# First group's routing spread between the search passes, its token slots one step later, and the second layer of its last slot moved into the second group's routing

## Chip, cores and metric

The program runs on one core of a Trainium2 chip. The metric is the device time of one execution in microseconds (us), lower is better.

## What is computed

Top-32 attention over 2 x 8 heads of 576 rows, then a mixture of eight experts (one expert for each token), then a dense mixture of four experts. The parts of the reference that matter:

```python
scores = scale * np.matmul(q, k.transpose(0, 1, 3, 2))
kth = np.partition(scores, -32, axis=-1)[..., -32:-31]
scores = np.where(scores >= kth, scores, -1000000000.0)      # then softmax
x = softmax(scores) @ v                                      # (1152, 512) after the heads are joined
logits = x @ w_gate + modality_bias[modality_id]
e_idx = np.argmax(logits, axis=1)                            # one expert of 8 for each token
out[mask] = gate_w[mask, None] * (np.maximum(x[mask] @ w1[e], 0.0) @ w2[e])
out2 += p[:, e:e + 1] * (np.maximum(x @ w1b[e], 0.0) @ w2b[e])   # four dense experts, all tokens
```

All of it is float32. Most products are done as three matmuls of rounded high and low parts.

## The kernel before

**Tiles and groups.** The 1152 tokens are 9 tiles of 128. A tile has 8 heads, so attention is 72 head steps (HEADS). Tiles 0 to 2 are the first group (GA), tiles 3 to 8 the second (GB). When the logits of a group are known, its tokens are sorted by expert into slots of 128 rows (at least one slot for each expert in use); each slot runs one expert's two layers. The slots of GA are worked during the attention of the later tiles, those of GB after attention. The four dense experts follow.

**Attention.** The program is one list of steps p = 0 to 77 on each engine, written out by hand. PE makes the scores of head p, multiplies attention by v for head p-6 (`att_times_v`) and transposes the attention of head p-5 (`transpose_att`). ACT copies scores, transposes and products out of PSUM and takes the exponential. POOL masks (`mask`, lines 656 and 659) heads 0 to 69, DVE the last two (line 1305). DVE finds the 32nd largest score of each row: for a pair of heads, 14 passes, that is two MAX8 on the scores (line 1093), then three rounds of two MATCH_REPLACE8 (line 1102) and two MAX8 (line 1107) (`find_thresholds`). After each pass it calls `pause()`, which takes one further piece of `work_beside` and moves DVE's clock on by 1/7 of a head.

**Routing.** `pick` finds each token's expert, `ranks` (PE) counts, `place` makes the tables: lines 1207 to 1271, about 30 small DVE instructions for GA, nine pieces between `yield`s. Inside a piece a helper `step` issues an instruction and waits for its semaphore before the next. `sum_tokens` (PE, line 1559) turns them into row numbers, by which POOL gathers the slots' rows. For GB the same pieces run in one go after attention; there the last tile is counted apart (`more_ranks`, lines 1551 and 1553, one tile at a time).

**GA's slots.** PE works slot s at steps A_START + 7s: `a_up` (first layer, line 1576), `a_turn` (transposes of the hidden values), `a_down` (second layer, line 1592), which reads `w2_raw`. Five slots (SPREAD) are in the list, from step 40; the fifth's second layer is at steps 73 and 74. SP loads weights (`a_load1`, `a_load2`), stores (`a_store`).

**First expert of GB.** Its number is known early (`turn_experts`, `spread_first` at step FIRST_AT = 66). SP loads its w1 into `w1_early`; ACT rounds it (`early_high`), POOL subtracts (`early_low`, line 672) at heads 67 to 70. Its w2 goes into `w2_raw` (`first_down`) after GA's fifth slot; ACT (`split_high`, line 885) and DVE (`split_low`, line 1279) split it.

**End of attention.** Step 77: the last two single counts, transposes of six heads of x (`x_most_transposes`), the last `att_times_v`; then `last_logits`, `pick_last`, `place(GB)`, `sum_tokens`, gather, `turn_slot(0)` (transpose of the gathered rows, line 1434), the register loads of the number of slots, `slot(0)`. A GB slot is 24 matmuls of layer one, three groups of four transposes, 24 matmuls of layer two (lines 1439 to 1441). After the last one DVE splits the first dense expert's w1 and copies the last slot's result (`copy_y`, line 1336), for which PE waits before `up_first`.

Each engine runs its own list in order. A wait holds everything behind it on that engine.

## Time and profile before

| | us |
|---|---|
| median of 3 runs | 920.28 (919.24 to 922.7) |
| the profiled execution | 921.51 |
| its span in the trace | 919.8 |

| engine | busy, us | share of the span |
|---|---|---|
| PE (matmul) | 860.4 | 94% |
| PE weight load | 724.1 | 79% |
| DVE | 551.2 | 60% |
| ACT | 341.1 | 37% |
| POOL | 295.5 | 32% |

The shares are means over stages with different limits. Times in the views are microseconds from the start of the span; a timeline row gives start, duration, engine, line of the kernel, operation, output and input, count, and in brackets the idle time ahead of it with what ended it. DVE is full to about 384 us, PE from about 417 us; between lies the end of attention and the second group's routing.

### The profile page before, as it was taken

Reading aid. Unit: us, or ns where it says so; the run is one execution under the profiler, and the core shown is the slowest. Engines: PE = TensorE matmul, PEld = TensorE weight load, DVE = VectorE, ACT = ScalarE, POOL = GpSimd, SP = SyncE. Lnnn points to the kernel's source line nnn. Section 1 sums busy time; section 2 is a strip of 40 time slices with the busy share of each in tenths; the row PEclk is TensorE's granted clock in tenths of the full one; section 3 lists DMA queues with packets and bytes.
Section 4 is the critical chain, followed back from the end, with each engine's and each line's share of the span. In section 5 each row is a group of like instructions: output and inputs, shape, how many; then the busy total and the mean of one; then the engine's idle time right before and its main releaser. Section 6 shows DMA issues by size and latency. Waiting matters only on the chain.

```text
span 919.8 us, 13596 instructions
## 1 busy us (share of the span) xinstructions
PE 860.4 (94%) x4895; PEld 724.1 (79%) x4895; DVE 551.2 (60%) x1087; ACT 341.1 (37%) x726; POOL 295.5 (32%) x243
## 2 busy tenths in 40 slices
PE   6799999948899999858999899999999999999998
PEld 5688888835566676646787789989898999899896
DVE  5999999999999999833482523414132422332121
ACT  5455556525465665431472412203130311222010
POOL 7876677547687666711110200000000000000000
PEclk9599999979899999868999999999999999999999
DMA  9320000024254355046193600112002200000001
GB/s 208 92 92 23 14 12 13 13 96 165 78 201 137 128 184 206 12 141 251 35 341 106 229 36 1 50 42 92 1 1 92 91 0 0 0 0 0 34 16 52
DMA packets 49394, 75.60 MB, mean 82 GB/s; under 512 B 24624, under 2 KB 24624, under 8 KB 49328
## 3 DMA queue, kind: packets, MB, share of 16 engines
q1 hardware_dynamic: 43088, 60.62, 19.4%
q0 software_dynamic: 4160, 13.63, 4.7%
q10 hardware_dynamic: 2080, 0.52, 0.3%
q8 instruction: 35, 0.57, 0.2%
q14 instruction: 31, 0.25, 0.1%
HBM read 63.49 MB, written 11.27 MB: 81 GB/s over the span
## 4 chain that ended last, share of the span: by engine, by line
PE 57%; DVE 38%; issue 4%; DMA 1%; ACT 1%; SPq 0%; DVEq 0%; POOLq 0%; ACTq 0%
PE bank L1439 17%; PE bank L1441 17%; PE bank L1440 17%; DVE work L1102 17%; DVE top L1107 13%; DVE top L1093 5%; PE bank L1434 2%; PE bank L1592 1%; PE bank L1495 1%; DMA k_raw<-in_k_dram 0%; DMA b_xs_raw<-x_dram,b_tok_i 0%; DVE b_hsTl L1349 0%; DVE kTl L1054 0%; PE bank L1466 0%; ACT b_hsTh L980 0%
## 5 line engine op out<-in xcount | busy, mean ns | idle before, releaser
L1107 DVE MAX8 top<-work 128x8 f32<-128x576 f32 x216 | 152.2, 743 | 0.1
L656 POOL TENSOR_SCALAR att<-sc,top 128x576 f32<-128x576 f32 x70 | 120.7, 1724 | 93.2 <-DVE top L1107 93.0
L1439 PE MATMUL bank<-xT,w1h 128*128 128x384 f32 x384 | 129.4, 337 | 3.4 <-DVE b_ys L1336 3.4
L1376 DVE SCALAR_TENSOR_TENSOR hT<-bank,hT 128x384 fp32r<-128x384 f32 x96 | 52.8, 557 | 131.0 <-ACT hT L1005 124.2
L1441 PE MATMUL bank<-xT,w1h 128*128 128x384 f32 x384 | 128.9, 336 | 0.0
L1440 PE MATMUL bank<-xT,w1l 128*128 128x384 f32 x384 | 128.9, 336 | 0.0
L1005 ACT ACTIVATE hT<-bank 128x384 fp32r<-128x384 f32 x96 | 46.9, 491 | 198.7 <-PE bank L1441 195.5
L1439 PE MATMUL bank<-w2h,hT 128*128 128x512 f32 x288 | 112.2, 390 | 1.2 <-DVE hT L1376 1.2
L1441 PE MATMUL bank<-w2l,hT 128*128 128x512 f32 x288 | 112.2, 390 | 0.0
L1440 PE MATMUL bank<-w2h,hT 128*128 128x512 f32 x288 | 112.2, 389 | 0.0
L1102 DVE MATCH_REPLACE8 work<-top,work 128x576 f32<-128x576 f32 x144 | 106.7, 746 | 0.0
L659 POOL TENSOR_TENSOR att<-att,ex 128x576 f32<-128x576 f32 x70 | 99.0, 1414 | 5.8
L1495 PE MATMUL bank<-v_one,attT 128*128 128x65 f32 (+1 forms) x800 | 93.3, 274 | 1.5 <-ACT av L805 1.3
L1495 PEld LDWEIGHTS bank<-v_one,attT 128*128 128x128 f32 (+1 forms) x800 | 85.9, 188 | 10.6 <-issue 7.2
L1388 DVE SCALAR_TENSOR_TENSOR x_tok<-bank,pr_e,x_tok 128x512 f32<-128x512 f32 x27 | 20.3, 751 | 115.0 <-PE bank L1441 115.0
L1439 PEld LDWEIGHTS bank<-xT,w1h 128*128 128x128 f32 x384 | 72.6, 189 | 4.1 <-issue 3.8
L1440 PEld LDWEIGHTS bank<-xT,w1l 128*128 128x128 f32 x384 | 72.6, 189 | 0.3
L1441 PEld LDWEIGHTS bank<-xT,w1h 128*128 128x128 f32 x384 | 72.5, 189 | 0.0
L797 ACT ACTIVATE attT<-bank 128x512 f32<-128x512 f32 x72 | 43.0, 597 | 79.7 <-PE bank L1466 78.0
L1605 PE MATMUL bank<-v_one 128*128 128x260 f32 x270 | 67.4, 397 | 0.0
L782 ACT ACTIVATE sc<-bank 128x576 f32<-128x576 f32 x72 | 46.4, 644 | 53.1 <-PE bank L1484 52.7
L1439 PEld LDWEIGHTS bank<-w2h,hT 128*128 128x128 f32 x288 | 54.1, 188 | 12.5 <-DVE hT L1376 1.5
(272 smaller groups left out, 1431.9 us busy)
## 6 DMA issues: line engine op xcount, KB each, us to landing
w_raw<-in_moe_w_dram SPq DMA_DIRECT2D x92, 512.0 KB, 6.0
q_raw<-in_q_dram SPq DMA_DIRECT2D x18, 128.0 KB, 2.9
v_one<-in_v_dram POOLq DMA_DIRECT2D x18, 128.0 KB, 4.9
out_dram<-x_tok SPq DMA_DIRECT2D x9, 256.0 KB, 2.0
y_dram<-zero POOLq DMA_DIRECT2D x2, 1024.0 KB, 6.7
w_early<-in_moe_w_dram SPq DMA_DIRECT2D x4, 512.0 KB
y_dram<-b_ys POOLq DMA_DIRECT2D x7, 256.0 KB, 2.6
k_raw<-in_k_dram SPq DMA_DIRECT2D x6, 256.0 KB, 4.8
```

The lines of the kernel that those rows point to most:

```text
L656: nc.gpsimd.tensor_scalar(att[:, g % ATR, :], sc[:, g % RING, :], top8[:, g % RING, 3, 7:8], None, ALU.is_ge).then_inc(keep_made, 1)
L659: nc.gpsimd.tensor_tensor(att[:, g % ATR, :], att[:, g % ATR, :], ex[:, g % EXR, :], ALU.mult).then_inc(att_made, 1)
L782: nc.scalar.activation(sc[:, g % RING:g % RING + 2, cols], bank[:, SB:SB + 2, 0:HS], ACT.Copy, scale=float(D) ** -0.5).then_inc(sc_copied, 1)
L1005: nc.scalar.activation(hTh(b)[:, f, :], bank[:, HB + f % 4, 0:BW], ACT.Relu).then_inc(h_high, 1)
L1102: nc.vector.match_replace(out=work[:, j, :], in_to_replace=top8[:, g % RING, i, :], in_values=sc[:, g % RING, :] if i == 0 else work[:, j, ...
L1107: nxt = nc.vector.max(out=top8[:, g % RING, i + 1, :], in_=work[:, j, :])
L1376: nc.vector.scalar_tensor_tensor(out=hTl(b)[:, f, :], in0=bank[:, HB + f % 4, 0:BW], scalar=0.0, in1=f32(hTh(b)[:, f, :]), op0=ALU.max, op ...
L1439: nc.tensor.matmul(dst, high_lhs, high_rhs, start=start, stop=False)
L1440: nc.tensor.matmul(dst, low_lhs, high_rhs, start=False, stop=False)
L1441: return nc.tensor.matmul(dst, high_lhs, low_rhs, start=False, stop=stop)
L1495: last = nc.tensor.matmul(bank[r0:r1, AVB, 0:W], attT[:, g % 2, c, r0:r1], v_one[b][:, h, c, :], start=(c == 0), stop=(c == KC - 1))
L1605: nc.tensor.matmul(bank[:, bk, 0:(KC - 1) * W], still[:, 0:P], moving, start=True, stop=True)
```

## The change

1. **GA's `place`** is cut into single instructions (or two that don't depend on each other) between the passes; `settle()` waits for the step before, one pass later. For GA the two int32 tables come straight from the reduction, without casts. A_START goes from 40 to 41, TOKENS_AT from 38 to 39. SP's first weight load no longer waits for the table.
2. **First expert of GB** is found ten steps earlier (from tile 3 alone); its `early_high` goes with slot 3 instead of 4, its `early_low` to heads 62, 63, 65, 66. `pick` for tiles 4 to 7 is one call between the two parts of the last division.
3. **End of attention:** the last head uses other PSUM banks (`head_banks`), so its transposes run ahead of the product of the head before; tile 7's transposes and logits are a step later; GB's counts go behind `last_logits` in one group, the last tile's in its own tensor `hot_last`.
4. **Second layer of GA's fifth slot:** its halves go behind `last_ranks` and behind `sum_tokens`. With it go ACT's `a_copy_y(4)` and SP's `a_store(4)`. `w2` for GB's first slot is loaded in two halves, each behind the half that frees `w2_raw`, and split in two halves, the second inside slot 0.
5. **GB slots:** the number of slots is loaded ahead of `turn_slot(0)`. In `slot` the transposes of the first hidden half go into the second half of layer one. At the end PE waits for the last `copy_y` behind `up_first`; DVE copies between the halves of the split.

```diff
-        RANKS_AT, TOKENS_AT, A_START, A_STEP, SPREAD = 36, 38, 40, 7, 5
+        RANKS_AT, TOKENS_AT, A_START, A_STEP, SPREAD = 36, 39, 41, 7, 5
-            ... p == t * H + (18, 18, 17, 22, 22, 22, 22, 17)[t]
+            ... p == t * H + (18, 18, 17, 22, 22, 22, 22, 18)[t]
-        FIRST_AT = HEADS - 6
+        FIRST_AT = HEADS - 16
+        EARLY = (62, 63, 65, 66)
+        def head_banks(g):
+            return (MB, SB + 1) if g == HEADS - 1 else (TBK, AVB)
 # SP
-                yield from clock.until(A_START + A_STEP * SPREAD)
-                a_store(SPREAD - 1)
+                yield from clock.until(1000)
+                keep_x(T - 1)
                 with sp.If(guarded(sp, GA, SPREAD)):
                     sp.sem_inc(passed, 1)
                 with sp.Else():
+                    sp.wait_ge(a_half_d, 1)
+                    first_down((0, 1))
                     sp.wait_ge(a_d, SPREAD)
-                    first_down()
-                yield from clock.until(1000)
-                keep_x(T - 1)
+                    first_down((2, 3))
+                a_store(SPREAD - 1)
 # POOL
-                if g >= HEADS - 1 - DC:
-                    early_low(g - HEADS + 1 + DC)
+                if g in EARLY:
+                    early_low(EARLY.index(g))
-            early_low(DC - 1)
 # ACT
-                yield from clock.until(A_START + A_STEP * SPREAD)
+                yield from clock.until(1000)
                 a_copy_y(SPREAD - 1)
...
-                if s >= 1:
-                    act.wait_ge(slot_y, s)
-                for i in range(2):
+                    if i == 0 and s >= 1:
+                        act.wait_ge(slot_y, s)
+                    if i == 1:
+                        slot_xT(s + 1)
                     act.wait_ge(slot_hT, 2 * s + i + 1)
-            split_high(0, w2_raw, w2h, w2_loaded, w2_high)
+            split_high(0, w2_raw, w2h, w2_loaded, w2_high, (0, 1))
             slot_xT(0)
 # DVE, place(): each step(...) becomes go(g, ...), yield, settle()
+                def settle():
+                    dve.wait_ge(g.route_step, g.steps)
-                step(nc.vector.tensor_scalar(g.counts[:, 1, :], total, 0.0, None, ALU.is_gt))
+                go(g, nc.vector.tensor_scalar(g.counts[:, 1, :], total, 0.0, None, ALU.is_gt))
+                yield
+                settle()
...
+                    if g is GA:
+                        with nc.allow_low_precision(reason="whole numbers below 100"):
+                            nc.vector.tensor_reduce(out=g.table_i[:, :, :], in_=g.cmp_pre[:, :, :, :], axis=AX.X, op=ALU.add).then_inc(g.experts_made, 1)
-                yield from place(GA, 1, clock.until(TOKENS_AT - 3.4))
-                yield from clock.until(FIRST_AT - 3)
-                yield from pick(GB, 0, GB.tiles - 3, 1)
+                yield from place(GA, 1, clock.until(TOKENS_AT - 2))
+                yield from clock.until(FIRST_AT - 5)
+                yield from pick(GB, 0, 1, 1)
             def last_slot(s):
-                split_low(ke, w1_raw, w1h, w1l, w1_high, w1_split)
+                split_low(ke, w1_raw, w1h, w1l, w1_high, w1_split, (0, 1))
                 copy_y(s - 1)
+                split_low(ke, w1_raw, w1h, w1l, w1_high, w1_split, (2, 3))
 # PE
+                    if s + 1 == SPREAD:
+                        break
                     yield from clock.until(at + 5)
                     a_down(s, (0, 1, 2, 3))
...
                 yield from clock.until(1000)
+                a_down(SPREAD - 1, (0, 1, 2, 3))
+                yield from clock.until(1001)
+                a_down(SPREAD - 1, (4, 5, 6, 7))
+                        if i == 1 and c == 2:
+                            if s >= 1:
+                                pe.wait_ge(slot_hT_split, 2 * s)
+                            turn_hidden(0)
...
             last_logits()
-            more_ranks(GB, GB.tiles - 1, 3)
+            pe.wait_ge(sc_copied, HEADS)
+            ranks(GB)
+            last_ranks()
+            clock.now = 1000
+            advance(work_beside)
             sum_tokens(GB)
-            clock.now = 1000
+            clock.now = 1001
             for _ in work_beside:
                 pass
-            turn_slot(0)
             pe.wait_ge(GB.table_made, 2)
...
+            turn_slot(0)
...
             pe.wait_ge(slot_hT_split, slots * 2)
-            pe.wait_ge(slot_y_copied, slots)
...
             up_first()
+            pe.wait_ge(slot_y_copied, slots)
```

## Rows read from the trace of the kernel before

**Rows 1.** Windows of all engines: start:end, length, busy us (PE PEld DVE ACT POOL), PE clock, DMA share, GB/s
```profile
350.00:371.00 21.00, 21.00 (x137) 14.89 (x136) 21.00 (x46) 13.17 (x31) 14.40 (x9) 1.00 0.62 226
376.00:383.00 7.00, 7.00 (x19) 3.89 (x19) 7.00 (x15) 3.27 (x8) 6.92 (x4) 0.62 0.01 2
416.60:422.30 5.70, 5.70 (x13) 4.45 (x14) 3.02 (x3) 0.18 (x1) 0.44 (x1) 0.50 1.01 390
514.70:517.80 3.10, 3.09 (x10) 3.09 (x11) 3.10 (x4) 0.57 (x1) 0.43 (x1) 0.50 0.83 251
```

**Rows 2.** The page: shares of the chain that ended last
```profile
PE 57%; DVE 38%; issue 4%; DMA 1%; ACT 1%; SPq 0%; DVEq 0%; POOLq 0%; ACTq 0%
```

**Rows 3.** Timeline of DVE, 185 to 200 us, first group's routing
```profile
185.29 0.74 DVE L1107 MAX8 top<-work 128x8 f32<-128x576 f32 x1
...
188.07 1.30 DVE L1217 CAST a_table_i<-a_table 128x18 int32<-128x18 f32 x1
...
197.02 0.17 DVE L1259 CAST a_by_slot_i<-a_by_slot 128x10 int32<-128x10 f32 x1
197.10 0.75 DVE L1107 MAX8 top<-work 128x8 f32<-128x576 f32 x1
...
199.32 0.09 DVE L1102 MATCH_VALUE_LOAD work<-top,work 128x8 f32 x1
```

**Rows 4.** Timeline of POOL in the same stretch
```profile
187.94 1.40 POOL L659 TENSOR_TENSOR att<-att,ex 128x576 f32<-128x576 f32 x1
```

**Rows 5.** Timeline of DVE, 383 to 399 us, end of attention
```profile
383.58 3.00 DVE L1305 SCALAR_TENSOR_TENSOR att<-sc,top,ex 128x576 f32<-128x576 f32 x1
386.79 0.82 DVE L1305 SCALAR_TENSOR_TENSOR att<-sc,top,ex 128x576 f32<-128x576 f32 x1 [0.21 <-DVE att L1305]
387.53 0.17 DVE L1160 TENSOR_TENSOR logits<-logits,bias_t 128x16 f32<-128x16 f32 x1
387.73 0.17 DVE L1161 TENSOR_REDUCE b_lmax<-logits 128x2 f32<-128x16 f32 x1
...
398.64 0.29 DVE L1135 TENSOR_TENSOR x_cur<-av,rden 128x128 f32<-128x128 f32 x1
```

**Rows 6.** Timeline of PE, 373 to 391 us
```profile
373.95 0.66 PE L1434 MATMUL bank<-ident,x_cur 128*128 128x128 f32 x4 [2.67 <-DVE x_cur L1135]
374.44 1.97 PE L1495 MATMUL bank<-v_one,attT 128*128 128x65 f32 x9
...
377.49 5.51 PE L1592 MATMUL bank<-w_raw,hsT 128*128 128x512 f32 x8
...
386.82 3.68 PE L1592 MATMUL bank<-w_raw,hsT 128*128 128x512 f32 x8
390.34 1.23 PE L1495 MATMUL bank<-v_one,attT 128*128 128x65 f32 x10
```

**Rows 7.** Timeline of POOL at the end of its masks
```profile
381.30 4.66 POOL L672 TENSOR_TENSOR w1l<-w_early,w1h 128x1024 fp32r<-128x1024 f32 x2
```

**Rows 8.** Timeline of PE, 406 to 417 us, second group's routing
```profile
406.51 1.45 PE L1559 MATMUL bank<-b_slot_token,b_row_hot 128*128 128x14 f32 x6 [4.08 <-DVE b_row_hot L1246]
...
412.61 1.12 PE L1434 MATMUL bank<-ident,b_xs_raw 128*128 128x128 f32 x4 [4.66 <-DMA b_xs_raw<-x_dram,b_tok_i]
...
416.60 0.79 PE L1439 MATMUL bank<-w1h,b_xsTh 128*128 128x512 f32 x1 [2.87 <-issue]
```

**Rows 9.** Timelines of PE in the second slot, then of ACT in the fifth
```profile
440.00 0.50 PE L1439 MATMUL bank<-w2h,b_hsTh 128*128 128x512 f32 x1 [0.57 <-DVE b_hsTl L1349]
...
475.38 1.06 ACT L885 ACTIVATE w2h<-w_raw 128x1024 fp32r<-128x1024 f32 x1 [0.17 <-DMA w_raw<-in_moe_w_dram]
```

**Rows 10.** Timeline of all engines between the slots and the dense experts
```profile
509.04 4.63 DVE L1279 TENSOR_TENSOR w1l<-w_raw,w1h 128x1024 fp32r<-128x1024 f32 x4 [2.31 <-ACT w1h L885]
...
513.58 0.68 DVE L1336 COPY b_ys<-bank 128x512 f32<-128x512 f32 x1
...
514.71 0.68 PE L1439 MATMUL bank<-xT,w1h 128*128 128x384 f32 x1 [3.38 <-DVE b_ys L1336]
```

More of the change, by code:

```diff
@@ L151, in routing_tensors @@
             g.cmp_slot = temps.take(f"{nm}_cmp_slot", [P, s, E])
+        hot_last = consts.take("hot_last", [P, E])
         routing_tensors(GA, consts)
@@ L484, in a_store, with load @@
                 sp.dma_start(y_a[s * P:(s + 1) * P, :], ys[:, :]).then_inc(a_stored, 16)
-            def load(e, kth, raw, src, split, loaded):
+            def load(e, kth, raw, src, split, loaded, parts=range(DC)):
                 sp.wait_ge(split, kth * DC + BASE)
@@ L489, in load @@
                 n = raw.shape[1] // DC
-                for c in range(DC):
+                for c in parts:
                     sp.dma_start(raw[:, c * n:(c + 1) * n, :], rows[:, c * n:(c + 1) * n, :]).then_inc(loaded[c], 16)
@@ L1208, in place @@
                                               jcol[:, 0:n].rearrange("p (o j) -> p o j", o=1).broadcast_to([P, E, n]), ALU.is_gt))
-                step(nc.vector.tensor_scalar(g.counts[:, 1, :], total, 0.0, None, ALU.is_gt))
-                step(nc.vector.tensor_reduce(out=g.counts[:, 0, :], in_=g.cmp_cnt[:, :, :], axis=AX.X, op=ALU.add))
-                step(nc.vector.tensor_tensor(g.cmp_pre[:, :, :, :], below[:, :, :].rearrange("p (o e) f -> p o e f", o=1).broadcast_to([P, 2, E + 1, E]),
+                go(g, nc.vector.tensor_scalar(g.counts[:, 1, :], total, 0.0, None, ALU.is_gt))
@@ L1212, in place @@
+                yield
+                settle()
+                go(g, nc.vector.tensor_reduce(out=g.counts[:, 0, :], in_=g.cmp_cnt[:, :, :], axis=AX.X, op=ALU.add))
+                yield
+                settle()
+                go(g, nc.vector.tensor_tensor(g.cmp_pre[:, :, :, :], below[:, :, :].rearrange("p (o e) f -> p o e f", o=1).broadcast_to([P, 2, E + 1, E]),
                                              g.counts[:, :, :].rearrange("p c (o f) -> p c o f", o=1).broadcast_to([P, 2, E + 1, E]), ALU.mult))
@@ L1222, in place @@
                 if g is GA:
-                    experts()
-                    nc.vector.tensor_copy(g.kth_expert_i[:, :], g.kth_expert[:, :]).then_inc(g.experts_made, 1)
+                    yield from experts()
                 yield
-                step(nc.vector.scalar_tensor_tensor(out=g.lg_a2[:, :, :], in0=over_t(g.table[:, 0, 0:E], n), scalar=float(P), in1=before_it, op0=ALU.mult, op1=ALU.add))
-                step(nc.vector.tensor_tensor(g.lg_a2[:, :, :], g.lg_a2[:, :, :], g.onehot[:, 0:n, :], ALU.mult))
@@ L1228, in place @@
-                step(nc.vector.tensor_reduce(out=g.pos_f[:, :], in_=g.lg_a2[:, :, :], axis=AX.X, op=ALU.add))
+                go(g, nc.vector.scalar_tensor_tensor(out=g.lg_a2[:, :, :], in0=over_t(g.table[:, 0, 0:E], n), scalar=float(P), in1=before_it, op0=ALU.mult, op1=ALU.add))
                 yield
+                settle()
+                go(g, nc.vector.tensor_tensor(g.lg_a2[:, :, :], g.lg_a2[:, :, :], g.onehot[:, 0:n, :], ALU.mult))
+                yield
+                settle()
+                go(g, nc.vector.tensor_reduce(out=g.pos_f[:, :], in_=g.lg_a2[:, :, :], axis=AX.X, op=ALU.add))
@@ L1316, in _ @@
             pick_last(GB)
-            for _ in place(GB, 4):
+            for _ in place(GB, 2):
                 pass
@@ L1546, in ranks, with last_ranks @@
                 last.then_inc(g.rank_made, 1)
-            def more_ranks(g, t, part):
-                n, rows = g.tiles, bank[:, g.rank_bank, :]
-                pe.wait_ge(g.hot_made, part)
-                nc.tensor.matmul(rows[:, t * E:(t + 1) * E], before[:, :], g.onehot[:, t, :], start=False, stop=False)
-                for u in range(t + 1, n + 1):
-                    last = nc.tensor.matmul(rows[:, u * E:(u + 1) * E], ones[:, :], g.onehot[:, t, :], start=False, stop=(t == n - 1))
-                last.then_inc(g.rank_made, 1)
+            def last_ranks():
+                n, rows = GB.tiles, bank[:, GB.rank_bank, :]
+                pe.wait_ge(GB.hot_made, 3)
+                nc.tensor.matmul(rows[:, (n - 1) * E:n * E], before[:, :], hot_last[:, :], start=False, stop=False)
+                nc.tensor.matmul(rows[:, n * E:(n + 1) * E], ones[:, :], hot_last[:, :], start=False, stop=True).then_inc(GB.rank_made, 1)
             def sum_tokens(g):
@@ L1685, in slot @@
                     last.then_inc(slot_h, 1)
-                if s >= 1:
-                    pe.wait_ge(slot_hT_split, 2 * s)
-                for i in range(2):
-                    pe.wait_ge(slot_relu, 2 * s + i + 1)
-                    transposes(HTB + i, lambda c: b_hs[:, (4 * i + c) * P:(4 * i + c + 1) * P]).then_inc(slot_hT, 1)
-                    if i == 0:
-                        turn_slot(s + 1)
+                turn_slot(s + 1)
+                turn_hidden(1)
                 if GA.tiles <= s < 2 * GA.tiles:
```

171 lines of the change are left out of this document (110 added, 61 removed).

## Prediction, made before the changed kernel was run

> **What bounds the kernel now.** I read the chain that ended last first: 38% of it is DVE and 57% PE [rows 2]. Then windows by stage: to 371 us DVE is busy in all of each window, and PE as well at the full clock [rows 1]. DVE sets the pace there, since its search passes follow each other without idle time, and the scores of the last pair were copied at 367.6 us, while DVE came to them at 373.8, so PE has some 6 us in hand. From the end of the search at 383.6 [rows 5] to the first GB slot at 416.60 [rows 8], 33 us, neither engine is full: the heads still in the pipeline, and the second group's routing. From 416.60 on PE is full but for short waits. So three kinds of time count: DVE time before 383, the chain of waits from 383 to 416, and holes of PE after it.
>
> **1. GA's routing on DVE.** From 185.29 to 199.32 are 14.03 us [rows 3]; in it lie six MAX8 at 0.66 us start to start and three MATCH_REPLACE8 with their value load at 0.72, together 6.1. The routing's 30 instructions take the other 7.9 us. An instruction that waits for the one before starts 0.20 us after it (387.53, then 387.73, duration 0.17) [rows 5]; one that doesn't wait starts 0.08 after (197.02, then 197.10, duration 0.17) [rows 3]. So a wait costs 0.12, and 19 of the steps lose theirs: 2.3 us. The other part is what POOL costs. The cast at 188.07 took 1.30 us instead of 0.17 and ended as POOL's multiply of 187.94 to 189.34 ended [rows 3, 4]; with four smaller ones I count 2.0 us of such waits in the 7.9. That cast becomes a reduction. But now the instructions lie over three pairs in which POOL masks steadily, not in a clump at which POOL ran dry: before, 17 small instructions beside a busy POOL lost 2.9 us, and without the cast's 1.1 that is 0.10 each, 2.9 for 30. So 2.3 + 2.0 - 2.9 = 1.4, and the two casts that go give 0.3: **1.7 us**. Bounds: 4.3 without any POOL wait; -3 if each waits twice as long as I take.
>
> The Trainium skill (SBUF — State Buffer, "SBUF: two separate sides") says that the read and write ports which DVE and GpSimd share are locked for a whole instruction, also against a DVE instruction with two SBUF inputs. By that rule spreading is a cost, and its reductions are safe. The cast row agrees; the third of POOL's time spent on two-input multiplies times 17 exposed instructions at 0.7 us gives an estimate of 4 us instead of 2.9, and the term would be 0.6.
>
> Tokens now come at DVE's step 37, so POOL waits with mask 35 for about 3 us. PE's first slot is a step later and PE has 6 us in hand; nothing is added.
>
> **2. End of attention.** The attention of head 70 took 3.00 us on DVE against 0.82 for head 71 [rows 5], while POOL ran its last two subtractions of w1 (381.30 to 385.96) [rows 7]. These now run at heads 62 to 66: 2.2 us less, head 71 is masked at 385.4 instead of 387.6. Before, PE then had a half of the second layer ahead of it (386.82, 3.68 us) and only at 390.34 took up head 69's product [rows 6]; the other half at 377.49 took 5.51 us at the low clock (1.2 GHz; mean 0.62 of the stretch) [rows 1, 6]. After, head 69's product is done by 381.7, and behind head 70's transposes at 384.45 come: transposes, tile 7's logits, head 71's transposes, product of 70, three transposes of x, product of 71. The product takes 1.23 us at the full clock and 1.97 at the low one [rows 6]. PE waits some 3 us before this, and before a wait of 2.67 us was followed by the low clock [rows 6]. So I take low: 1.1 + 1.2 + 1.1 + 2.0 + 0.8 + 2.0 = 8.2, ending at 392.65; a copy and three small DVE steps make x whole at 393.65. Before it was whole at 398.93 [rows 5]. **5.3 us**; with the sum at the full clock (5.2) 8.3.
>
> **3. Second group's routing.** GB's counts (14 matmuls, 1.5 us) move behind the last logits, beside DVE's `pick_last` of 1 us: tables start 0.75 us later against x. So `row_hot` is ready at 406.5 - 4.55 = 401.9. In front of `sum_tokens` stands now the first half of the second layer, from 397.9; at the low clock it takes 5.3 us, to 403.2. Sum to 404.6 (before 407.96 [rows 8]), so the lead is 3.3. The second half takes 3.7 (clock up again by then, as before at 383 after 6 us of dense work [rows 1, 6]) to 408.3. Behind it stand a branch with its register load (1.1) and two register loads: three took 2.87 us ahead of 416.60 [rows 8], so 1.9: PE is free at 411.3. The gather starts at 405.8 and took 3.5 us, to 409.3, or 1 more beside the load of w2. Now ACT: it copies y at 408.4, branches, then rounds w2's first half, loaded from 403.7 (2 x 512 KB, by 410), at 1.04 us each [rows 9], to 412.05, and only then the slot's rows (0.6); DVE 0.7: **slot 0 starts at 413.4 instead of 416.60**. Of 5.3 us 3.2 are left, so this part costs 2.1. Cheapest: the loads of the registers hidden and no second layer in the way, a gain of 1.4 more. Dearest: w2's half lands after 9.6 us (the slowest weight load in the trace), ACT has it at 415.9 and slot 0 starts at 417.2, a loss of 5.9. Queued behind the wait for the second layer: on ACT the rounding and the slot's rows, on SP the second half of w2 and y's store, on POOL three gathers of x, all needed by 420 at the earliest.
>
> The first layer of slot 0 still runs 5.7 us at half clock [rows 1].
>
> **4. In the slots.** Before, PE waits 0.57 us ahead of the second layer [rows 9]. After, only the second hidden half is awaited, with `turn_slot` beside it: 0.3 less in four slots, 1.2 together. But where an expert changes, ACT is busy with w2: its last chunk ends at 476.4 [rows 9], then the relu takes 0.6, to 476.95, while PE now wants it at 475.85 in the middle of layer one; a loss of 1.0 there and 0.5 in the slot before, 0.1 in the sixth. Net **-0.4**, between -1.6 and 1.2.
>
> **5. Slots to dense.** PE waited 3.38 us, for DVE's `copy_y` behind the whole split of w1 [rows 10], and then ran 3.1 us at half clock [rows 1]. Now the first chunk (split at 510.3) is all it needs, and PE makes 2.05 us of matmuls from each chunk of 1.15. **3.4 us**. If PE too needs time for the branch, as DVE with 2.31 idle [rows 10], 1.1; if the clock stays up, 3.1 x 0.5 = 1.5 more, 4.9.
>
> The rest has one answer: w1 of the first expert arrives a good 20 us before its use, its rounding finds ACT at 60% busy, `hot_last` and the banks add one copy of 0.2 us that hides beside the counts.
>
> **Sum.** 1.7 + 5.3 - 2.1 - 0.4 + 3.4 = 7.9 us. The profiled execution would go from 921.5 to 913.6. It was 1.2 above the median of the three runs; on the median's scale 920.3 - 7.9 = **912.4 us**.
>
> **Rivals.**
> - *The clock stays up.* Dense work at 397.9 to 408 and fewer holes could keep PE at 2.4 GHz: 3.0 more in part 2, and slot 0's first layer without 5.7 us at half clock, 2.9 more. 920.3 - 13.8 = 906.5. For it: the hole of part 5 goes. Against: PE waits again some 5 us ahead of slot 0, as before [rows 1, 8].
> - *Waits on DVE are free.* The 0.12 is then no cost of the wait but of the operand, and part 1 is 2.3 less: 914.7. The Trainium skill says so (VectorE: DVE Perf Modes, "The DRAIN you can't avoid"): a semaphore after each of eight copies cost nothing. The spacings 0.20 and 0.08 speak against it here [rows 3, 5].
> - *The second layer is only moved.* It fills no hole, but lengthens the chain to slot 0: low clock in both halves (5.3 + 5.3) and w2's half late. Slot 0 at 417.2, part 3 costs 5.9: 916.2.
> - *Slower: the port.* Each spread instruction waits for POOL. The price is up to 1.13 us [rows 3]; 17 exposed ones make 19 us, part 1 is -15 and the time 929. It decides from 0.6 us on each exposed one, when part 1 eats the other 6.2. Against it: of 17 instructions before only two waited over half a microsecond.
>
> **How the numbers follow.** Forecast 0.45; clock up 0.2; waits free 0.1; only moved 0.15; port 0.05; something that I don't see 0.05. The range from **905.5 to 917.5** takes in the first four with the bounds of part 4 and 5 and leaves out the port and half of the rest. A measurement of this kernel can tell 0.5% (4.6 us) from no change: faster is below 915.7, which holds the forecast, the clock and waits free, mostly, and a third of only moved: 0.77. Same 0.17, slower 0.06.
>
> **What would show it.** Part 1: from the first routing instruction of GA to the last some 38 us instead of 13, but the pair (70, 71) starts at about 372 instead of 373.8. Part 2: att of head 70 in 0.82 us; x whole about 10 us after the last search pass instead of 15.4; clock 0.5 there. Part 3: the L1592 groups at about 396 and 403 (with part 1's gain), `sum_tokens` directly behind the first, ACT's rounding as the last thing ahead of slot 0. Part 4: a PE wait in the middle of layer one in slots 3 and 4. Part 5: no wait at L1439 behind the last slot. I am wrong if the last pair starts later than 373.8, if the lead at slot 0 is under 2 us or above 8, or if a new wait shows between the slots.

## The result, and the profile after

| | before | after |
|---|---|---|
| median, us | 921.21 (5 runs, 919.24 to 924.39) | 914.49 (5 runs, 913.67 to 915.15) |
| profiled execution, us | 921.51 | 913.67 |
| its span, us | 919.8 | 911.9 |

The ratio of after to before is 0.9931, interval 0.9906 to 0.9956: the change gives 6.7 us, where 7.9 were forecast. The two profiled executions differ by 7.9 us of span, but 2.3 of these belong to neither kernel: the first search pass began at 14.35 us after and at 16.63 before, because the first scores came sooner, and the same start varies between 14.2 and 16.6 us among the runs of this study (15.96 in e7, which is the kernel before up to there). I therefore compare stages, each from its own beginning (read from the timelines of DVE and PE). The search is DVE's passes for the thresholds and ends with its last MAX8. x is whole when DVE has written the last part of `x_cur`. Slot 0 starts with its first matmul of layer one, and the dense experts with their first:

| stage, us | before | after | gain | forecast |
|---|---|---|---|---|
| pair 32 to pair 38 (GA's routing) | 39.21 | 36.52 | 2.7 | |
| pair 38 to the end of the search | 169.46 | 171.15 | -1.7 | |
| both | 208.67 | 207.67 | 1.0 | 1.7 |
| end of the search to x whole | 15.38 | 10.64 | 4.7 | 5.3 |
| x whole to slot 0 | 17.67 | 21.89 | -4.2 | -2.1 |
| slot 0 to the dense experts | 98.11 | 95.44 | 2.7 | 3.0 |
| dense experts to the end | 405.04 | 403.65 | 1.4 | 0 |
| sum | | | 5.6 | 7.9 |

The windows of the kernel after, as in [rows 1] (start:end, length, busy us of PE PEld DVE ACT POOL, PE clock, DMA share, GB/s). The third is new, the first half of the moved second layer with the counts before it:

```profile
350.00:371.00 21.00, 20.62 (x118) 13.52 (x116) 21.00 (x43) 11.16 (x31) 18.77 (x12) 1.00 0.35 113
376.00:383.00 7.00, 4.72 (x24) 4.36 (x24) 5.91 (x11) 1.99 (x6) 0.00 (x0) 0.61 0.01 2
396.00:400.40 4.40, 4.40 (x9) 2.33 (x9) 3.37 (x15) 0.00 (x0) 0.00 (x0) 0.50 0.00 0
412.81:418.50 5.69, 5.69 (x13) 4.47 (x14) 2.21 (x2) 0.16 (x1) 1.96 (x3) 0.50 0.37 118
508.20:511.30 3.10, 3.05 (x17) 3.05 (x18) 3.10 (x4) 3.10 (x4) 0.57 (x1) 1.00 0.22 90
```

DVE is still full to the end of the search. Slot 0's first layer still starts at half clock (fourth row), and the first dense matmuls now run at the full clock (fifth row; 0.50 in [rows 1]). The chain that ended last, which was [rows 2], now runs over PE for most of the span:

```profile
PE 70%; DVE 21%; POOL 3%; issue 2%; ACT 2%; DMA 1%; SPq 0%; DVEq 0%; ACTq 0%; POOLq 0%
```

**DVE in the search.** The timeline of DVE after, answering [rows 3], then where the second group's first expert is named, ten heads earlier than before:

```profile
187.08 0.28 DVE L1241 TENSOR_REDUCE a_table_i<-a_cmp_pre 128x18 int32<-128x144 f32 x1
187.29 0.61 DVE L1244 TENSOR_TENSOR a_cmp_kth<-a_table,ecol 128x64 f32<-128x64 f32 x1
...
198.75 1.00 DVE L1308 TENSOR_SCALAR a_by_slot_i<-a_by_slot 128x10 int32<-128x10 f32 x1
...
299.10 0.17 DVE L1194 TENSOR_SCALAR turned_by<-turned_less 128x8 f32<-128x8 f32 x1
299.30 1.26 DVE L1195 TENSOR_TENSOR turned_less<-turned_less,turned_by 128x8 f32<-128x8 f32 x1
```

POOL's timeline at the same place:

```profile
299.12 1.42 POOL L670 TENSOR_TENSOR att<-att,ex 128x576 f32<-128x576 f32 x1
```

The cast of 1.30 us is a reduction of 0.28. But an instruction on 128x8 took 1.26 us and ended as POOL's mask ended (300.56 and 300.54), as the cast did in [rows 3, 4]. From pair 46 to 60 the kernel after needs 71.86 us and the one before 67.77; later it gets 2.4 of these back (60.44 and 62.85 us to the end; 62.15 in e7, so 1.7 to 2.4), where the pieces stood before.

**From the search to slot 0.** DVE, to set beside [rows 5]:

```profile
380.31 0.82 DVE L1365 SCALAR_TENSOR_TENSOR att<-sc,top,ex 128x576 f32<-128x576 f32 x1
...
390.63 0.29 DVE L1146 TENSOR_TENSOR x_cur<-av,rden 128x128 f32<-128x128 f32 x1
```

PE, to set beside [rows 6, 8]:

```profile
377.70 2.37 PE L1563 MATMUL bank<-v_one,attT 128*128 128x65 f32 x10 [1.07 <-ACT av L816]
381.28 0.44 PE L1531 MATMUL bank<-ident,att 128*128 128x128 f32 x1 [1.21 <-DVE att L1365]
...
393.11 2.69 PE L1613 MATMUL bank<-b_onehot,ones 128*128 128x48 f32 x12
...
396.51 6.12 PE L1658 MATMUL bank<-w_raw,hsT 128*128 128x512 f32 x8
402.06 1.13 PE L1625 MATMUL bank<-b_slot_token,b_row_hot 128*128 128x14 f32 x6
403.05 3.68 PE L1658 MATMUL bank<-w_raw,hsT 128*128 128x512 f32 x8
410.74 0.66 PE L1497 MATMUL bank<-ident,b_xs_raw 128*128 128x128 f32 x4 [4.02 <-DMA b_xs_raw<-x_dram,b_tok_i]
412.81 0.80 PE L1502 MATMUL bank<-w1h,b_xsTh 128*128 128x512 f32 x1 [1.41 <-DVE b_xsTl L1382]
```

ACT and POOL in the same stretch:

```profile
408.17 2.00 ACT L896 ACTIVATE w2h<-w_raw 128x1024 fp32r<-128x1024 f32 x2 [0.81 <-issue]
411.44 0.60 ACT L971 ACTIVATE b_xsTh<-bank 128x512 fp32r<-128x512 f32 x1 [1.27 <-PE bank L1497]
```

```profile
404.32 1.05 POOL L728 DMA_INDIRECT b_xs_raw<-x_dram,b_tok_i  x1 [28.56 <-DVE b_pos_i L1272]
```

The attention of head 70 takes 0.82 us as forecast. The last thing ahead of slot 0 is not ACT's rounding (done at 410.17) but the gather: issued at 404.32, its rows reach PE at 410.74. That is 6.42 us, where the kernel before needed 3.5.

**Slots and dense.** PE in slot 3, and at the join that [rows 10] showed with 3.38 us of waiting:

```profile
459.00 0.63 PE L1497 MATMUL bank<-ident,b_hs 128*128 128x128 f32 x4 [0.49 <-ACT b_hs L985]
...
508.25 0.44 PE L1502 MATMUL bank<-xT,w1h 128*128 128x384 f32 x1 [0.18 <-issue]
```

### The profile page after: what moved, and what is told of

Same layout as the page of the kernel before. It is cut to its first block, busy times and chain, and to the rows that moved or that the text cites. A ratio compares the mean times of both kernels' runs of the same rounds, so it can differ in the third digit from the quotient of the medians.

```text
span 911.9 us, 13566 instructions
## 1 busy us (share of the span) xinstructions
PE 862.8 (95%) x4885; PEld 725.5 (80%) x4885; DVE 550.0 (60%) x1087; ACT 341.7 (37%) x726; POOL 296.4 (33%) x243
## 4 chain that ended last, share of the span: by engine, by line
PE 70%; DVE 21%; POOL 3%; issue 2%; ACT 2%; DMA 1%; SPq 0%; DVEq 0%; ACTq 0%; POOLq 0%
PE bank L1502 17%; PE bank L1504 17%; PE bank L1503 17%; DVE work L1113 10%; DVE top L1118 7%; PE bank L1673 6%; PE bank L1563 5%; DVE top L1104 3%; PE bank L1551 2%; PE bank L1497 2%; PE bank L1533 2%; POOL v_one L628 1%; ACT w2h L896 1%; DMA b_xs_raw<-x_dram,b_tok_i 1%; PE bank L1658 1%
## 5 line engine op out<-in xcount | busy, mean ns | idle before, releaser
L1563 PE MATMUL bank<-v_one,attT 128*128 128x65 f32 (+1 forms) x800 | 96.3, 281 | 2.2 <-ACT av L816 2.1
L1563 PEld LDWEIGHTS bank<-v_one,attT 128*128 128x128 f32 (+1 forms) x800 | 88.8, 195 | 11.8 <-issue 7.7
```

The costliest lines, as they stand in the source:

```text
L1563: last = nc.tensor.matmul(bank[r0:r1, sums, 0:W], attT[:, g % 2, c, r0:r1], v_one[b][:, h, c, :], start=(c == 0), stop=(c == KC - 1))
```

## Experiments

My theory was the sum on record. Open were: what a wait on DVE costs and what POOL does to the spread instructions; what the clock does in the drain, that is while the last heads pass through the pipeline; which wait ends last ahead of slot 0; and whether the new order inside the slots pays. A time of one execution says little: the ten of e7 lie within 5.7 us and the six of e9 within 2.3. So I compare stages. They too come from one execution each and mostly repeat within 0.1 us, but not always. Programs that are alike up to there differ by 0.6 us from pair 32 to 38 (35.94 in e11 and 35.95 in e9, 36.5 in the others), by 0.7 from pair 32 to the end of the search (208.67 before, 208.00 in e7), and by 1.2 from x whole to slot 0 (20.82 to 22.07 in after, e1, e2, e8, e11). A smaller difference in these stages shows nothing.

### The waits of the first group's routing

`e1_wait_at_once`: each wait stands directly behind its instruction again, one instruction for each pass as in the change. `e2_clumped`: the same, and several instructions in one gap between passes, in groups much as before.

```diff
                 go(g, nc.vector.tensor_scalar(g.counts[:, 1, :], total, 0.0, None, ALU.is_gt))
-                yield
                 settle()
+                yield            # e2: left out but for four places
```

> The changed kernel with one thing turned round: in GA's routing on DVE each instruction is still put alone between two search passes, but its wait stands directly behind it and not behind the next search pass. Same places, same instructions. Read from the start of the pair of heads 32 to the start of pair 38 (36.52 us after, 39.21 before). If a wait costs 0.12 us each: 19 of them, so 36.5 + 2.3 = 38.8. If waits on DVE are free (the rival): 36.5. In the whole time 2 us more or none.

> The changed kernel with GA's routing put back into its old pieces (nine, each with a wait behind every step); the two casts stay reductions and the token slots stay a step later. Pair 32 to pair 38: if the waits are the whole gain of part 1, 38.8 as in the run with waits at once. If spreading exposes the instructions to POOL as I took it (0.10 each), the pieces meet it less: 37.5 to 38.3. If the gain came from the pieces themselves, 39 or more.

Measured from pair 32 to 38: before 39.21, e2 38.95, e1 37.81, after 36.52 us. The rest of the search is untouched (46 to 60 is 71.84 and 71.85). So the gain of 2.7 splits into 0.26 for the casts (too little to be told from none), 1.14 for the spreading alone, and 1.29 for the waits, 0.07 each. There are 18 of them in `place(GA)`, not 19. A wait is not free. The 0.07 is a net value: the small instructions of this stretch last 8.95 us in all in e1 and 9.65 after, so POOL held them 0.7 us less in e1, and a wait by itself may cost up to 0.11. The part that I took for a cost, the spreading, is a gain (the small instructions last 10.31 us in e2): in e2's clump POOL's masks still met instructions, for one this row of DVE in e2 (the same instruction takes 0.18 us after):

```profile
189.19 1.02 DVE L1270 TENSOR_TENSOR a_cmp_row<-a_pos_f,jcol 128x33 f32<-128x33 f32 x1
```

### The second group's first expert off POOL's masks

`e3_off_the_masks` moves both its pieces a little later, to where POOL waits for the next thresholds; `e10_naming_alone` and `e11_pick_alone` move one each.

```diff
-                yield from clock.until(FIRST_AT)
+                yield from clock.until(FIRST_AT + 1.55)
-                yield from clock.until(FIRST_AT - 5)
+                yield from clock.until(FIRST_AT - 4.7)
```

> The changed kernel with the two pieces of DVE work that find GB's first expert moved by a few search passes, into the stretch of a pair in which POOL has finished its masks: the pick of tile 3 from DVE's step 51 to 51.3, the naming from 56 to 57.55. In the changed kernel these pieces lengthen their pairs by 1.33 and 2.76 us, 4.09 together. If POOL's masks cause the excess (each instruction takes 0.17 when alone): 2.1 together, the end of the search 2 us earlier. If it has another cause (the wait for PE's or ACT's word): 4.1 as before.

> Only one of the two moves: the naming of the second group's first expert 1.55 heads later, its pick stays where it is. The stretch from pair 46 to pair 60 should be 1.5 us shorter (of the 2.05 of both), 70.4. The clock tells two theories apart. If the clock falls in the drain because DVE's search is late against the heads, this one has most of that gain and stays at 1.00 to 384 us, with x whole 6.7 us after the search. If it was chance, it may as well be 0.50 from 378 us on, with x whole after 10.6.

> Only the other move: the pick for the second group's first expert 0.3 of a head later, its naming stays. Pair 46 to 60: 0.5 us shorter, 71.3. Clock: theory 'late search' says 0.50 from about 378 us and x whole 10.6 us after the search, as in the changed kernel, since nearly nothing is gained; theory 'chance' allows either.

| | after | e3 | e10 | e11 |
|---|---|---|---|---|
| pair 46 to 60, us | 71.86 | 69.81 | 70.08 | 71.55 |
| pair 32 to the end of the search | 207.67 | 206.78 | 207.18 | 206.79 |
| end of the search to x whole | 10.64 | 6.69 | 6.68 | 10.65 |
| one execution, us | 914.49 (median) | 906.97 | 907.58 | 914.20 |

e11's 206.79 holds 0.6 us gained in pairs 32 to 38, which its edit does not touch. DVE's naming in e10, with the instruction that took 1.26 us at 299.30:

```profile
306.53 0.17 DVE L1194 TENSOR_SCALAR turned_by<-turned_less 128x8 f32<-128x8 f32 x1
306.74 0.17 DVE L1195 TENSOR_TENSOR turned_less<-turned_less,turned_by 128x8 f32<-128x8 f32 x1
```

So 2.05 us of part 1 were lost to POOL's masks in these two places. In e3 only 0.9 of them, in e10 0.5 of 1.8, arrive at the end of the search, since DVE now waits for scores. Its timeline in e10:

```profile
328.52 1.42 DVE L1104 MAX8 top<-sc 128x8 f32<-128x576 f32 x2 [0.53 <-ACT sc L792]
...
339.30 1.42 DVE L1104 MAX8 top<-sc 128x8 f32<-128x576 f32 x2 [1.04 <-ACT sc L792]
```

The kernel after has no wait of DVE there. The larger gain was one that e3 did not aim at: PE kept the full clock through the drain, and x is whole 4 us sooner. Windows of PE in e10:

```profile
376.00:380.00 4.00, 2.74 (x24) 1.00 0.00 0
380.00:384.00 4.00, 4.00 (x39) 1.00 0.02 4
```

PE's timeline shows the other difference. In e10 PE is held at 302 us by the naming, which it hadn't waited for:

```profile
306.32 1.09 PE L1497 MATMUL bank<-ident,q_high 128*128 128x128 f32 x4 [3.96 <-DVE first_less L1190]
```

From there to the end of attention its heads run later, which I take to be what made DVE wait for the scores: head 67's product starts at 373.85 us in e10 and at 371.25 after. So the wait of 1.21 us ahead of head 70's transposes (381.28, above) does not occur. Holding PE also costs clock where it is held: the low stretch there lasts 6.8 us in e10 (305.9 to 312.7) and 3.4 after (312.7 to 316.1).

### Is it PE's lateness?

`e12_one_more_wait` takes the changed kernel and adds one wait on PE. DVE's list stays as it is.

```diff
+                if p == FIRST_AT + 1:
+                    pe.wait_ge(top_step, 5 * FIRST_AT + 6)
                 if high is not None:
                     q_transposes(high, "qh")
```

> The changed kernel with nothing but one wait more on PE: at step 57, ahead of a group of transposes, PE waits until DVE has made the second round of replacements of pair 56 (about 306.2 us), as it waits for DVE's naming at 306.3 in the kernel with the naming alone. DVE's list is untouched, so pair 46 to 60 stays 71.9 and the end of the search stays at 207.7 after pair 32. My theory of why the clock stayed up with the late naming: PE was held 4 us at 302, so its heads ran about 2.3 us later to the end and the waits ahead of head 70's transposes (1.1 to 1.2 us of them) closed; then the same happens here: PE at 1.00 to 384 us, x whole 6.7 us after the search instead of 10.6, slot 0 20.5 us behind it instead of 21.9, in all 5 us less, 909.5, by a wait that was added. The rival says that it is DVE's gained time (the search ends earlier against PE's work of the slots) and not PE's lateness: then PE is at 0.50 from 378 us on, x whole comes after 10.6, and the time is 914.5 or up to 1 us more.

I put it too early in PE's list: PE came to it at 294 us instead of 302 and stood for 13.5 us, which then starved the search (pair 46 to 60 80.04 us instead of 71.86). The time, 918.92 us (10 runs, ratio to before 0.9988, 0.9967 to 1.0009), is no gain. The rival is answered all the same, since the search here lost 9.3 us and gained nothing, and yet the clock stayed up in the profiled execution. The other nine executions had mean granted clocks of 0.954 to 0.957 against 0.959 in the profiled one, so it is not shown that they kept it too. PE's wait, then two windows around the end of the search (391.4):

```profile
307.90 2.39 PE L1563 MATMUL bank<-v_one,attT 128*128 128x65 f32 x10 [13.50 <-DVE work L1113]
```

```profile
387.50:391.50 4.00, 2.75 (x24) 2.33 (x23) 3.96 (x9) 3.80 (x11) 0.00 (x0) 1.00 0.00 0
391.50:395.50 4.00, 4.00 (x38) 4.00 (x39) 2.79 (x7) 2.00 (x7) 0.00 (x0) 1.00 0.01 4
```

x whole came 6.67 us after the search. The profiles built on the changed kernel without fillers fall into two groups. Where PE also waits ahead of head 70's transposes (1.2 to 2.3 us, beside earlier waits of 0.63, 0.19 and 1.07), the clock is 0.50 in the whole of 384 to 388 and x whole takes 10.6 us (after, e1, e2, e4, e5, e8, e11). Where it doesn't, the clock is 1.00 until x is whole and that takes 6.7 (e3, e9, e10, e12).

But this wait cannot be what lowered the clock in all of the first group. In the kernel after it lasts from 380.07 to 381.28, and the clock had fallen at 377.53. Windows of PE after:

```profile
375.00:377.50 2.50, 1.54 (x13) 1.00 0.00 0
377.70:380.00 2.30, 2.30 (x10) 0.50 0.00 0
```

In e2, e4 and e5 too the fall comes before this wait. In e1, e8 and e11 it comes 0.2 to 1.7 us after its start, as in these windows of e8 (its wait began at 379.27):

```profile
376.90:380.90 4.00, 1.30 (x11) 1.00 0.00 0
381.10:385.00 3.90, 3.46 (x17) 0.50 0.02 4
```

So the wait marks the profiles in which PE was early, and which part of PE's idle time in 370 to 381 us lowered the clock was not separated. What is shown is that the same two waits of 0.63 and 1.07 us went with a fall in some profiles and not in others, and that PE later against the search went with none.

### Filling the hole

`e6_filled` keeps PE busy in it with 24 unread matmuls (128x128).

```diff
+                if p == AV_END - 2:
+                    unread(MB + 2, 18)
                 if 0 <= p - TR_LAG < HEADS and p != AV_END - 1:
                     transpose_att(p - TR_LAG)
+                if p == AV_END - 3:
+                    pe.wait_ge(a_ys, SPREAD - 1)
+                    unread(MB + 2, 6)
```

> The changed kernel with 24 matmuls of 128 columns whose result nobody reads put into PE's two waits at the end of attention (6 ahead of head 69's product, 18 behind it), 2.6 us of work at the full clock. In the changed kernel the clock falls at 377.7 and stays at 1.2 GHz until 403. If PE's idle time there is the cause: the clock stays at 2.4 GHz through the last heads, x is whole 3 us earlier (10.6 us behind the last search pass becomes 7.6), the 14 count matmuls take 1.6 instead of 3.0 us, the first half of the second layer 3.7 instead of 5.6; slot 0 starts 3 to 6 us earlier. If the chain there is bound by ACT's and DVE's copies: x is whole at most 1 us earlier.

Measured: 910.99 us, one execution; clock 1.00 from 370 to 388. So with the two waits filled the clock did not fall. (PE was also 1.4 us later in this execution before the first filler: head 67's product starts at 372.68 instead of 371.25. In e11, where PE stood about as late, the clock fell.) x whole comes 9.17 us after the search: 1.5 less than after, and 2.5 more than in e10, which is what the fillers themselves delay. They took 1.5 and 4.2 us where I had reckoned 2.6 in all, and PE comes to head 70's transposes 2.6 us later against the search than after. The rest of the expectation failed: the clock fell again at 390.75, so the counts still took 3.6 us and the half of the second layer 5.0. x whole to slot 0 takes 20.81 instead of 21.89, which is within what this stage varies by.

### Ahead of slot 0

`e4_sum_first` puts `sum_tokens` ahead of the first half of the second layer. `e5_gather_first` keeps the order of PE, but SP loads the second layer of slot 0 only when the slot's rows have landed, and ACT rounds those rows first.

```diff
# e4, PE
+            sum_tokens(GB)
             clock.now = 1000
             advance(work_beside)
-            sum_tokens(GB)
# e5, SP, then ACT
+                    sp.wait_ge(slot_loaded[0], 16)
                     sp.wait_ge(a_half_d, 1)
-            split_high(0, w2_raw, w2h, w2_loaded, w2_high, (0, 1))
             slot_xT(0)
+            split_high(0, w2_raw, w2h, w2_loaded, w2_high, (0, 1))
```

> The changed kernel with both halves of the second layer of GA's fifth slot behind the sum of the tokens instead of one half ahead of it. In the changed kernel the first half ends at 402.1 and the sum waits for it, though DVE's table was ready at 400.7. If the half ahead is what makes the gather late: sum 1.4 us earlier, gather issued at 402.9 (on the scale of the changed kernel's trace) instead of 404.3; but w2's first half is loaded 3 us later, behind the gather, so the gather lands after 3.5 us instead of 6.4, and ACT has w2 rounded only at about 414: slot 0 starts 1 to 2 us later than 412.8. If w2 is not what ACT waits for: slot 0 up to 4 us earlier.

> The changed kernel with SP's load of w2 held back until the first gathered rows have landed, and with ACT taking slot 0's rows before it rounds w2. In the changed kernel the gather took 6.4 us from issue to landing beside the load of w2, before 3.5 us alone. If the load beside it is the cause: 3.5 us again, slot 0 starts 2.5 to 3 us earlier than 412.8, and its second layer waits for w2 at most 1 us. If the gather is slow for another reason (x stored late, the queue): 6 us as now, and no gain.

| | before | after | e4 | e5 |
|---|---|---|---|---|
| x whole to the gather's issue, us | 10.16 | 13.40 | 12.38 | 13.42 |
| issue to PE's transposes of the rows | 3.52 | 6.42 | 8.75 | 4.40 |
| x whole to slot 0 | 17.67 | 21.89 | 24.28 | 19.88 |

PE, then ACT in e4:

```profile
402.12 8.47 PE L1658 MATMUL bank<-w_raw,hsT 128*128 128x512 f32 x16
412.15 0.66 PE L1497 MATMUL bank<-ident,b_xs_raw 128*128 128x128 f32 x4 [1.55 <-issue]
```

```profile
413.94 0.58 ACT L971 ACTIVATE b_xsTh<-bank 128x512 fp32r<-128x512 f32 x1
```

In e4 the gather is issued 1.0 us sooner, but the whole second layer (8.47 us) then stands on PE between it and its use, and ACT has the result of that layer and w2 to do ahead of the rows: 2.4 us worse. In e5 the gather needs 4.40 instead of 6.42 us and slot 0 starts 2.0 us sooner; the rounding of w2 starts at 414.99, in the shade of layer one, and the gain is still there at the dense experts (x whole to dense 115.10 against 117.33). How much of the 4.2 us the loads beside the gather cost is known roughly: with the loads beside it the same gather took 4.75 (e6) to 6.4 us in nine profiles, held back 4.40 (e5) and 4.71 (e9). From x whole to slot 0, e5 is 0.9 to 2.2 us below after, e1, e2, e8 and e11, and e9 1.6 to 2.3 below e3, e10 and e12, where the clock was up as well. So holding back the loads gives some 1 to 2 us.

### The last part alone, and the old order in the slots

`e7_last_part_alone` is the kernel before with part 5 of the change only; `e8_old_slots` is the changed kernel with the old order of transposes in `slot`.

```diff
# e7, PE
-            pe.wait_ge(slot_y_copied, slots)
             up_first()
+            pe.wait_ge(slot_y_copied, slots)
# e7, DVE
-                split_low(ke, w1_raw, w1h, w1l, w1_high, w1_split)
+                split_low(ke, w1_raw, w1h, w1l, w1_high, w1_split, (0, 1))
                 copy_y(s - 1)
+                split_low(ke, w1_raw, w1h, w1l, w1_high, w1_split, (2, 3))
# e8, PE
-                        if i == 1 and c == 2:
-                            turn_hidden(0)
...
+                turn_hidden(0)
                 turn_slot(s + 1)
                 turn_hidden(1)
```

> The kernel before with one piece of the change alone: PE waits for the last slot's copied result behind the first dense layer and not ahead of it, and DVE makes that copy between the halves of the split of w1. Before, PE waited 3.38 us here and then ran 3.1 us at half clock. Expected: no wait at L1439 behind the last slot, the clock stays at full, 3.4 + 1.4 = 4.8 us less, 915.5 to 916.5, ratio 0.995. If PE also pays for leaving the nest of branches, as DVE does with 2.3 us: 1.1 less only. If the time is given back later (w2's split is not earlier): nothing.

> The changed kernel with the old order inside a GB slot: both groups of hidden transposes behind the first layer, ACT and PE as before. In the changed kernel the seven slots take 95.26 us from the first matmul of slot 0 to the last of slot 6, before 94.57. If the group in the middle of the first layer costs where an expert changes (slots 3 and 4, 0.5 and 1.0 us by my sum) and gives 0.3 elsewhere: 94.6 to 95.0 here. If the slots are longer for another reason (w2 in two halves): 95.3 still.

e7: 915.04 us (10 runs; ratio to before 0.9947, 0.9925 to 0.9969). Slot 0 to dense 94.01 instead of 98.11, dense to the end 403.65 instead of 405.04. This small part of the change gives 4.9 us (2.9 to 6.9 by the interval) where the whole gives 6.7. Its window behind the slots:

```profile
510.00:513.00 3.00, 3.00 (x19) 3.00 (x18) 3.00 (x4) 3.00 (x4) 0.57 (x1) 1.00 0.21 87
```

e8: 912.76 us, one execution; slot 0 to dense 94.59 instead of 95.44, all stages up to x whole as after. This difference by itself proves little, since the stage holds the end of a low clock of changing length and takes 94.83 to 95.66 in profiles with the same order (e10, e12). I therefore take half of the time at low clock off the length of the seven slots (first matmul of slot 0 to the last of slot 6), an estimate from the clock's two levels. With the old order this leaves 91.9 us before (94.73 with 5.69 at low clock; not 94.57, as the expectation has it), and 91.8 in e7, e8 and e9. With the new order it leaves 92.3 to 92.5 in eight profiles, among them after (95.26 with 5.68), 92.8 in e6 and 93.1 in e5. The groups do not overlap: the new order costs some 0.6 us. Only 0.1 of it is waiting: PE's idle times in the seven slots add up to 2.98 us after and 2.88 before. The rest lies in PE's busy time, and its cause was not separated.

### Three together

`e9_three_together` has the edits of e3, e5 and e8.

> The changed kernel with three edits together: the second group's first expert found a little later, beside POOL's subtractions instead of its masks; the gather of slot 0's rows ahead of the rounding and of the load of its second layer; the old order inside the slots. Single edits gave, against the changed kernel: 0.9 us less to the end of the search and 4.0 less from there to x whole (full clock); 2.0 less from x whole to slot 0; 0.5 to 0.85 less from slot 0 to the dense experts. Theory 'they add, and the clock stays up because of the late expert': 914.5 - 0.9 - 4.0 - 1.4 - 0.7 = 907.5, all runs within 1.5 us of one another. Theory 'the clock was luck of that one execution': 914.5 - 0.9 - 1.4 - 0.7 = 911.5, with PE at 0.50 from about 378 us in the profile; if it is luck in each execution, times scattered over the 4 us between. Rival, nothing adds (each gain only moves the wait to another engine): 913 or more.

903.72 us (6 runs, 902.92 to 905.2; ratio to before 0.9831, 0.9804 to 0.9858). That is 10.8 us below the changed kernel and below both theories; the executions lie within 2.3 us, and all have a mean granted clock of 0.962 to 0.964, so the clock was no luck of one execution. Against after, by stages: search 1.1 (0.6 of it in pairs 32 to 38, which no edit touches), to x whole 3.9, to slot 0 3.4, slot 0 to dense 2.0 less. Of the 3.8 us below the 907.5, 2.0 are e5's, which I had left out of the sum, and 1.3 came between slot 0 and the dense experts, where 0.7 was counted: the low clock lasts 3.4 us there instead of 5.7. PE and then a window of slot 0's start:

```profile
402.38 0.66 PE L1499 MATMUL bank<-ident,b_xs_raw 128*128 128x128 f32 x4 [2.31 <-DMA b_xs_raw<-x_dram,b_tok_i]
```

```profile
404.44:408.40 3.96, 3.96 (x10) 3.12 (x11) 0.24 (x1) 1.15 (x2) 0.00 (x0) 0.57 0.97 310
```

PE waits 2.31 us instead of 4.02 for the rows, and its half clock in slot 0 ends 3.9 us after the slot's start instead of 5.7.

## Why the prediction was right, and where its steps were off

**Part 1** (forecast 1.7, measured 1.0, or 0.3 with e7's search in place of that of the kernel before). The term of GA's routing was 1.7 and measured 2.7, and two of its parts were wrong in opposite directions. The wait was priced at 0.12 by the spacings of [rows 3, 5] and cost 0.07 net (e1), for 18 waits instead of 19. The spreading was booked as 0.9 lost to POOL and gained 1.1 (e2 against e1). What I put under "the rest has one answer", naming the second group's first expert earlier, cost 1.7 to 2.4 net: the row of 1.26 us shows an instruction held by a POOL mask, and e3 takes 2.05 us of it away by moving the pieces out of the masks. So [rows 3, 4] held the warning, and I applied it to the wrong group of instructions. The rival *waits on DVE are free* falls by e1: 1.29 us for 18 waits, twice what the stage varies by in the same program. The rule of the Trainium skill behind it (VectorE: DVE Perf Modes, "The DRAIN you can't avoid") says of a semaphore behind each of eight copies that it costs nothing; for the small instructions here e1 disagrees with 0.07 us for each. The rival *the port* is real in single places (1.26 and 1.00 us above) but not for each spread instruction.

**Part 2** (5.3, measured 4.7). The low clock was right, and the attention of head 70 is 0.82 us as worked out. The other branch was undersized: 3.0 more was forecast for a clock that stays up, e10 and e12 show 4.0. I gave that branch 0.2 and argued for the low clock by a wait of some 3 us ahead of head 70's transposes. That wait is 1.2 us, and the clock had fallen 2.5 us before it began, so the level was right and its reason was not; what lowered it stays open within PE's idle time of 370 to 381 us.

**Part 3** (-2.1, measured -4.2). Two terms were mis-sized. GB's counts were taken at 1.5 us and take 4.0 at the low clock (392.67 to 396.65; the trace has 18, not 14), so `row_hot` came 9.75 us after x whole instead of 8.25. The gather was taken at 3.5, or 1 more beside w2, and took 6.4, of which e5 and e9 put some 1 to 2 down to the load beside it. So the path was wrong as well: it was to run over ACT's rounding of w2, and it ran over the gather. Against these, the register loads, counted at 1.9, stood in the shade of the gather and cost nothing, and w2's rounding was done 1.3 us before ACT had rows to round. The halves of the second layer started at 396.51 and 403.05, close to the 396 and 403 on record, but by luck: the search began 2.3 us earlier in this trace, and counted from x whole they came at 5.6 and 12.1 us instead of 4.3 and 11.0. *The second layer is only moved* put slot 0 23.6 us behind x whole and the forecast 19.8; 21.89 lies half way, but the mechanism of that rival, low clock in both halves and w2's half too late, did not occur (the second half took 3.68 us).

**Part 4** (-0.4, measured -0.5 in the profiled pair; -0.6 by the slots of all profiles). Four waits of 0.56 to 0.61 us ahead of the second layer became 0.25, the 0.3 less of the forecast, and the waits in the middle of layer one show where they were expected, at a change of expert (459.00, 0.49 us). But all waits together changed by 0.1 us and not by 0.4, and some 0.5 us more of busy PE, for which the sum had no term, makes up the number. The size was right partly by luck.

**Part 5** (3.4, measured 3.2 and 1.4 more). The wait went, and so did the half clock behind it, which I had at 1.5 as the upper bound. With no hole in front of it there was no fall: the 4.9 of the other branch was the better value, and e7 measures it.

Together 5.6 in the profiled pair and 6.7 between the medians against 7.9; the 1.1 between the two is not explained. The total is closer than its parts: part 5 gave back 1.2 of the 3.5 that parts 1 to 4 were over. One of the prediction's own signs of being wrong came true, a lead at slot 0 under 2 us. The traces differ there by 3.8 us (416.60 and 412.81), but 2.3 of these are the earlier start, and parts 1 to 3 leave 1.5 of the 4.9 forecast. The measured 914.49 is also next to the 914.7 of *waits on DVE are free*, whose mechanism e1 refutes; the time alone could not have told them apart.

## What to carry to other kernels

Price a small instruction on DVE by what POOL does at the same moment, not by its own length: moved beside POOL's waits instead of its masks, the same pieces cost 2.05 us less. Where an engine's clock falls in a hole, compare the time of the fall with the time of each wait before naming one as the cause. Holding PE earlier, where it has time in hand, went with a clock that stayed up later (here at the price of 1.6 us in which DVE waited for scores), and a wait removed at a join gives its own length and the slow matmuls behind it. Here it paid to let a small gather on the critical path land before large loads were started beside it.

## What the runs showed of the hardware that I had not expected

- Whether PE kept its clock at the end of attention went with how PE stood against the search. With 3.96 us of waiting at 302 us and no wait at 380, PE ran at 2.4 GHz through the drain (e10), and with 13.5 us of waiting at 294 as well (e12). The changed kernel ran there at 1.2 GHz from 377.53 us on.
- One gather of a slot's rows took 3.5 us in the kernel before and in e7, 4.4 and 4.7 with the weight loads held back (e5, e9), and 4.75 to 6.4 with them beside it (nine profiles).
- Casts and one-input instructions were held by POOL like two-input ones: the cast of [rows 3] took 1.30 us, and TENSOR_SCALAR on 128x10 1.00 us (198.75 after) and ended as POOL's mask ended; on 128x14, where POOL masked nothing, it took 0.17 (404.61).
